# Which units' results stay in PSUM, where a softmax chunk ends, and GpSimd's order, in the first iteration of an attention and two-FFN kernel

## What is computed

```
w = exp(weight_gen - max) / (sum + 1e-9)              # softmax over the 7 taps
x1[b,s,h,g] = sum over k of w[b,s,h,k] * x[b,s-6+k,h,g]  # causal window of 7 tokens
h1 = x1 @ w_in1 ; g1 = h1 * cos(h1) ; x2 = g1 @ w_out1
h2 = x2 @ w_in2 ; g2 = max(0.01*h2, h2) ; out = g2 @ w_out2
```

## Time and profile before

| | |
|---|---|
| median of 3 executions | 1163.77 us |
| lowest and highest | 1163.77 and 1166.3 us |
| the profiled execution's own time | 1166.25 us |
| its span | 1164.4 us |
| TensorE matmul busy | 1146.1 us (98%) |
| VectorE, ScalarE, GpSimd busy | 900.9, 735.9, 84.9 us |
| granted TensorE clock, mean | 0.997 of full |

### The profile page before, as it was taken

The page is one execution under the profiler, slowest core; times in us unless marked ns, Lnnn a source line. Parts: engine busy times, 40 slices in busy tenths (PEclk is TensorE's granted clock), DMA queues, the critical chain, the costliest instruction groups (busy, mean ns, idle before and its releaser), DMA issues.

```text
span 1164.4 us, 23292 instructions
## 1 busy us (share of the span) xinstructions
PE 1146.1 (98%) x10170; PEld 950.1 (82%) x10170; DVE 900.9 (77%) x862; ACT 735.9 (63%) x804; POOL 84.9 (7%) x81
## 2 busy tenths in 40 slices
PE   7889999999999999999999999999999999999998
PEld 5768888888888888888888888888888888888876
DVE  8878797878879788697786868868697886968433
ACT  5666674766657676575755747566575655757554
POOL 5850000000000000000000000000000000000000
PEclk9999999999999999999999999999999999999999
DMA  9760101001010000101001010000101001000000
GB/s 260 202 120 1 35 1 49 1 2 49 1 49 1 20 30 1 49 1 49 1 2 48 1 48 1 22 28 1 48 2 49 1 1 48 1 15 1 15 1 28
DMA packets 20653, 37.40 MB, mean 32 GB/s; under 512 B 5196, under 2 KB 14794, under 8 KB 20168
## 3 DMA queue, kind: packets, MB, share of 16 engines
q1 hardware_dynamic: 16104, 30.66, 8.4%
q0 software_dynamic: 4448, 5.24, 2.5%
HBM read 29.61 MB, written 6.29 MB: 31 GB/s over the span
## 4 chain that ended last, share of the span: by engine, by line
PE 92%; DVE 2%; SPq 2%; POOL 2%; ACT 1%; issue 1%; DMA 1%; ACTq 0%; POOLq 0%
PE slot L1064 43%; PE acc_a L1064 28%; PE acc_b L1064 19%; DMA x_win<-in_x 1%; DVE g_lo L825 1%; POOL prods L307 1%; POOL prods L298 1%; SPq L463 0%; DVE prods L307 0%; POOL out_hi_lo L554 0%; PE slot L1009 0%; DVE gate L897 0%; PE acc_b L1037 0%; PE slot L996 0%; ACT g_hi L637 0%
## 5 line engine op out<-in xcount | busy, mean ns | idle before, releaser
L1064 PE MATMUL acc_a<-g_hi,out_hi_lo 64*128 64x512 f32 x2000 | 697.5, 389 | 0.0
L1064 PEld LDWEIGHTS acc_a<-g_hi,out_hi_lo 64*128 64x128 f32 x2000 | 369.0, 184 | 36.8
L825 DVE TENSOR_TENSOR g_lo<-gate,g_hi 128x1024 fp32r<-128x1024 f32 x248 | 303.6, 1224 | 117.5 <-ACT g_hi L637 116.9
L1064 PE MATMUL acc_b<-g_hi,out_hi_lo 64*128 64x512 f32 x1000 | 389.1, 389 | 1.6 <-DVE g_lo L825 1.5
L1064 PE MATMUL acc_b<-g_lo,out_hi_lo 64*128 64x512 f32 x1000 | 387.5, 387 | 0.0
L1064 PE MATMUL acc_a<-g_lo,out_hi_lo 64*128 64x512 f32 x1000 | 387.3, 387 | 0.0
L637 ACT ACTIVATE g_hi<-gate 128x1024 fp32r<-128x1024 f32 x248 | 262.9, 1060 | 94.3 <-PE acc_b L1064 77.5
L1064 PE MATMUL slot<-x_a_hi,in_a_lo 64*128 64x512 f32 x1024 | 299.6, 394 | 5.2 <-DVE g_lo L825 2.5
L1064 PE MATMUL slot<-x_b,in_b_hi 64*128 64x512 f32 x1024 | 296.4, 388 | 0.2 <-DVE x_b L839 0.2
L1064 PE MATMUL slot<-x_a_lo,in_a_hi 64*128 64x512 f32 x1024 | 296.3, 387 | 0.0
L1064 PE MATMUL slot<-x_a_hi,in_a_hi 64*128 64x512 f32 x1024 | 296.2, 387 | 0.0
(11 more groups left out here) (100 smaller groups left out, 1073.9 us busy)
## 6 DMA issues: line engine op xcount, KB each, us to landing
x_win<-in_x SPq DMA_DIRECT2D x14, 960.0 KB, 4.7
out<-result SPq DMA_DIRECT2D x16, 384.0 KB, 2.3
out_raw<-in_moe_w_out SPq DMA_DIRECT2D x3, 512.0 KB, 8.5
out_hi_lo<-in_moe_w_out POOLq DMA_DIRECT2D x2, 768.0 KB, 11.0
out_hi_lo<-in_moe_w_out POOLq DMA_DIRECT2D x1, 1536.0 KB, 14.5
taps_w<-in_weight_gen SPq DMA_DIRECT2D x2, 560.0 KB, 9.4
in_a_raw<-in_moe_w_in SPq DMA_DIRECT2D x1, 1024.0 KB, 5.3
out_raw<-in_moe_w_out SPq DMA_DIRECT2D x1, 1024.0 KB, 11.6
```

What stands on the lines that cost most here:

```text
L825: nc.vector.tensor_tensor(g_lo[:, q % 2, :], result_of(i - b, q), g_hi[:, q % 2, :].bitcast(FP32), ALU.subtract)\
L1064: return nc.tensor.matmul(to, w[rows, :], x[rows, :], start=start, stop=stop)
```

## The change

Three things change, all but one detail in iteration 0.

1. `stays` is true for units 2, 3 and 4 of iteration 0 alone. Units 0, 1, 5, 6 and 7 put their product into `gate`, and their slot is free once the product is done.
2. The softmax of chunks 1 and 2 keeps a common max, subtract and exp. The sum, guard, invert and multiply are done for chunk 1 alone ahead of unit 0, and for chunk 2 after step 9 of iteration 0, in half-size instructions. The load of the sine table moves from step 14 to 12.
3. GpSimd's `out_lows(2)` comes ahead of the first pair addition rather than behind it. VectorE's split of chunk 1's input comes after the fraction of unit 7, not ahead of it.

```diff
     def stays(i, q):
-        return i == 0 and q < len(FIRST_UNITS)
+        return i == 0 and q in (2, 3, 4)
...
-        SOFT_CHUNKS = [(0, 1), (1, 3), (3, 6), (6, 11), (11, C)]
+        SOFT_HEADS = [(0, 1), (1, 3), (3, 6), (6, 11), (11, C)]
+        SOFT_CHUNKS = [(0, 1), (1, 2), (2, 3), (3, 6), (6, 11), (11, C)]
...
-        EXP_STEP, SINE_STEP = 10, 14
+        EXP_STEP, SINE_STEP = 10, 12
...
+        SOFT_AT = {(0, 9): [(2, part) for part in TAIL_PARTS]}
...
             out_lows(1)
-            of_pool[2]()
             out_lows(2)
-            for instruction in of_pool[3:]:
+            for instruction in of_pool[2:]:
                 instruction()
...
-                if step == FIRST_INPUT_SPLIT and input_splits(i, step):
-                    split_low(FIRST_INPUT_STEP, i + 1)
                 if in_first and i == 0 and step == FIRST_UNITS[0]:
...
+                if step == FIRST_INPUT_SPLIT and input_splits(i, step):
+                    split_low(FIRST_INPUT_STEP, i + 1)
                 pending_low(i, step)
...
-                    if unit(j, UNITS.index(s)) == 0:
-                        pe.wait_ge(unit_dve, 3)
                     pe.wait_ge(lo_ready, unit(j, UNITS.index(s)) + 1)
                 elif what == "first":
+                    if unit(j, UNITS.index(s)) == 0:
+                        pe.wait_ge(unit_dve, 2)
                     pe.wait_ge(g_ready, first_units(j, UNITS.index(s)))
```

More of the change, by code:

```diff
@@ L275, in window_attention_two_ffn @@
         ATT_STEPS = 11
-        SOFT_CHUNKS = [(0, 1), (1, 3), (3, 6), (6, 11), (11, C)]
+        SOFT_HEADS = [(0, 1), (1, 3), (3, 6), (6, 11), (11, C)]
+        SOFT_CHUNKS = [(0, 1), (1, 2), (2, 3), (3, 6), (6, 11), (11, C)]
+        HEAD_OF = [n for a, _ in SOFT_CHUNKS for n, (b, e) in enumerate(SOFT_HEADS) if b <= a < e]
         ATT_MULTS = 9
-        SOFT_PARTS = ["max", "subtract", "sum", "guard", "invert", "multiply"]
-        SOFT_ORDER = [(n, part) for n in range(len(SOFT_CHUNKS)) for part in SOFT_PARTS]
+        HEAD_PARTS, TAIL_PARTS = ["max", "subtract"], ["sum", "guard", "invert", "multiply"]
+        SOFT_ORDER = []
+        for n, head in enumerate(HEAD_OF):
+            if head not in HEAD_OF[:n]:
+                SOFT_ORDER += [(head, part) for part in HEAD_PARTS]
+            SOFT_ORDER += [(n, part) for part in TAIL_PARTS]
         def soft_count(n, part):
@@ L399, in first_lows @@
                    b_pairs(W1.in_b_hi, cols).bitcast(FP32))
[L401 to L405 removed]
+        EXP_STEP, SINE_STEP = 10, 12
+        HEAD_ROWS, SOFT_ROWS = [[slice(a * J * heads, b * J * heads) for a, b in chunks]
+                                for chunks in (SOFT_HEADS, SOFT_CHUNKS)]
+        SOFT_AT = {(0, 9): [(2, part) for part in TAIL_PARTS]}
         for n, (begin, end) in enumerate(((1, 1), (2, 3), (4, 5)), 2):
@@ L408, in window_attention_two_ffn, with softmax_operands @@
             SOFT_AT.setdefault((begin, 8 if n == 2 else 14), []).append((n, "subtract"))
-            SOFT_AT[end, 13] = [(n, "sum")]
-            SOFT_AT[end, 14] = [(n, "guard"), (n, "invert")]
-            SOFT_AT[end, 16] = [(n, "multiply")]
+            SOFT_AT[end, 13] = [(n + 1, "sum")]
+            SOFT_AT[end, 14] = [(n + 1, "guard"), (n + 1, "invert")]
+            SOFT_AT[end, 16] = [(n + 1, "multiply")]
         EXP_AT, SINE_AT = [[(i, step) for i in (1, 3, 5)] for step in (EXP_STEP, SINE_STEP)]
-        def softmax_operands(n):
-            rows = SOFT_ROWS[n]
+        def softmax_operands(rows):
             part = taps_w[:, rows, :]
@@ L442, in load_gen @@
             def load_gen(n):
-                rows = SOFT_ROWS[n]
+                rows = HEAD_ROWS[n]
                 sp.dma_start(taps_w[:, rows, :], gen_rows[:, rows, :]).then_inc(gen_loaded[n], 16)
@@ L912, in step_of @@
                         dve.wait_ge(ready, n)
-                        nc.vector.scalar_tensor_tensor(slot[:, cols], slot[:, cols], RADIANS,
+                        nc.vector.scalar_tensor_tensor(result_of(i, q)[:, cols], slot[:, cols], RADIANS,
                                                        gate[:, 0, cols], ALU.mult, ALU.mult)\
@@ L934, in softmax @@
             def softmax(n, part):
-                rows = SOFT_ROWS[n]
+                rows = (HEAD_ROWS if part in HEAD_PARTS else SOFT_ROWS)[n]
                 weights, sums = taps_w[:, rows, :], scratch[:, rows]
@@ L941, in softmax @@
                     dve.wait_ge(soft, soft_count(n, "max"))
-                    ins = nc.vector.tensor_tensor(*softmax_operands(n), ALU.subtract)
+                    ins = nc.vector.tensor_tensor(*softmax_operands(rows), ALU.subtract)
                 elif part == "sum":
-                    dve.wait_ge(exp_ready, n + 1)
+                    dve.wait_ge(exp_ready, HEAD_OF[n] + 1)
                     ins = nc.vector.tensor_reduce(sums, weights, AX.X, ALU.add)
@@ L953, in softmax @@
                     dve.wait_ge(soft, soft_count(n, "invert"))
-                    ins = nc.vector.tensor_tensor(*softmax_operands(n), ALU.mult)
+                    ins = nc.vector.tensor_tensor(*softmax_operands(rows), ALU.mult)
                 ins.then_inc(soft, 1)
-            for part in SOFT_PARTS:
+            for part in HEAD_PARTS + TAIL_PARTS:
                 softmax(0, part)
@@ L963, in _ @@
                 nc.vector.tensor_tensor(lo, raw, hi, ALU.subtract).then_inc(w1_first_lo, 1)
-            for part in SOFT_PARTS[:2]:
+            for part in HEAD_PARTS:
                 softmax(1, part)
             split_low(INPUT_STEP, 0)
-            for part in SOFT_PARTS[2:]:
+            for part in TAIL_PARTS:
                 softmax(1, part)
```

8 lines of the change are left out of this document (4 added, 4 removed).

## The result

The changed kernel takes 1167.89 us (median of 11, 1166.77 to 1169.21) against 1165.14 us for the kernel before (11 runs, 1163.77 to 1166.58): ratio 1.0025, 95% interval 1.0016 to 1.0034. Timed again (run 1) it was 1167.91 against 1165.94 us, 1.002 (1.001 to 1.0029). So it is 2 to 3 us slower. The forecast was 1164.4 us and the range ended at 1167.3: missed.

A forecast was written before the change was run, and what follows sets the result against it. TensorE, busy 98% of the span, was taken as the bound, with only the first 80 us mattering. Terms +0.6 + 0.3 - 0.3 = +0.6 us on 1163.77 gave 1164.4 us, range 1159.3 to 1167.3.

The forecast's parts named there:

- the 0.3 us wait: TensorE's wait after 110 us, which loading the sine table at step 12 should take away: 0.3 us gained.
- the four waits: TensorE's waits of 2.38, 1.16, 2.48 and 1.23 us in the first 80 us; with slow stretches 10.7 us at most.
- Turns by whole instructions: VectorE and GpSimd: an instruction with two SBUF inputs waits for the other engine's running one, then precedes its next.
- rival 2: GpSimd's w_in2 instructions only stretch chunk 2's softmax tail, to 2.7 us in all: 1161.3 us, chance 0.25.
- Part 1: Fewer units stay in iteration 0: unit 0's fraction 1.06 us earlier; after its both_products the kernel 2.3 us ahead.
- GpSimd's chain: GpSimd's work from 29.72 us to chunk 1's attention: pair addition at 40.4, attention's end at 54.1, 0.4 us later.
- the reordering: out_lows(2) ahead of the first pair addition: would use 2.59 us of GpSimd idling, but VectorE's added turns eat it.
- part 2: Chunk 2's softmax tail after unit 7's low part: costs 5.1 us; iteration 1's first unit's sum 0.6 us behind.
- The rule on waits: TensorE: only waits over 2 us bring a slow stretch at 1.2 GHz, costing 1.7 us each.
- Rival 4: Held-up tail plus slow stretches behind unit 2's slot, unit 5's sum and the 2.5 us wait: 1167.8 us, chance 0.10.
- The base: The time before to which the forecast change of +0.6 us was added: the median, 1163.77 us, not the profiled 1166.25.

The follow-up runs named there:

- run 3: Changed kernel, but GpSimd starts its work on w_in2 only when the multiply of chunk 2's softmax is done: 1163.82 us, ratio 0.9989 to the kernel before.
- run 7: Changed kernel with out_lows(2) back behind the first pair addition and chunk 2's softmax tail after step 5 of iteration 1: 1164.49 us, ratio 0.9984.
- run 5: Changed kernel with 5 and 7 useless matmuls in TensorE's two waits ahead of the sum of iteration 1's first unit: 1166.24 us, ratio 0.9998.
- run 11: Kernel before with chunk 2's softmax ended after step 9 of iteration 0, sine table at step 12, split behind unit 7's fraction: 1164.23 us, ratio 0.9982.
- run 2: Changed kernel with chunk 2's softmax tail moved from after step 9 of iteration 0 to after step 5 of iteration 1: 1162.85 us, ratio 0.9978.

## Why the prediction was wrong

**What bounds the kernel.** Right: after 110 us nothing differs but the 0.3 us wait, which went as forecast (with it 0.5 us, counted from the fold on). One reading was wrong: the first of the four waits, which ends at 31.43 us with unit 0's low part, can't have the attention's end at 53.7 behind it; only the last three can.

**Turns by whole instructions.** Right, and run 3 shows it: 0.18 and 0.39 us against 1.97 and 2.13 with the same VectorE list. The rule of the Trainium skill (SBUF — State Buffer, Who interferes with whom) that the loser blocks for the full instruction is what the guard and the multiply do against instructions of 2.4 us, and the trace agrees: they end at 67.10 and 69.65 us, within 0.3 us of GpSimd's second and third instruction. The stretching of rival 2 would have made the tail 2.7 us long, and it was 4.9.

**Part 1 and GpSimd's chain.** The order of events was as worked out, at each step about 1 us earlier: pair addition 39.4 (forecast 40.4), attention's end 53.3 (54.1), unit 6's low part 61.2 (62.2), end of the tail 69.65 (70.9), the sum 76.56 (77.7). That VectorE's turns eat the reordering was half right: run 7 gives the order 1 us beside them. The 2.3 us by which the kernel was to be ahead were 3.0 (the first both_products of iteration 1 is over at 64.76 instead of 67.79), but they were worth nothing, since they only brought TensorE earlier to a wait whose end VectorE sets.

**The step that failed** is the last one of part 2: "so a slow stretch comes, but most of it lies under the wait for the low part; 0.3 us is left." It was 1.65 us in the first profile and 2.4 to 2.6 in the second, the median execution. The stretch did not begin with the fill after the first wait, as I had assumed, so that the second wait would cover it; it began at the end of the second wait (76.5 us) or within it (75.4), and nearly all of it fell on work. Runs 1 and 5 show its length and its price.

**The rule on waits** (only over 2 us) was too simple: two waits of 1.79 and 1.74 us with 1.4 us of work between them bring a stretch; a wait of 2.34 us has one behind it in the first profile of the changed kernel and none in the second. A pair of waits isn't needed either: single ones of 1.79 us (run 5) and 1.91 us (run 11, ahead of unit 3's fill) had a stretch behind them, and ones of 1.85 (run 3) and 1.87 us (run 11, ahead of the transpose) had none. So the length of the wait alone doesn't decide it, and what does is open. Rival 4 had the right mechanism for the last of its three stretches, at a price of 4 us in all and a chance of 0.10; of its other two, the one behind unit 2's slot never came and the one behind unit 5's sum came in one profile of two. A good part of it should have stood in the forecast.

**The base.** The time was forecast on the lowest of the three runs shown as median, though the profiled execution was 2.5 us above it. With 35 runs of before from 1163.37 to 1168.54 us (median 1165.94), a profile at 1166.25 is nearly the median, and the forecast should have been tied to it: 1166.85. That the first profiled execution of the changed kernel took just 1166.83 us would have been luck: its sum came 1.1 us earlier than forecast, and its stretch cost 1.3 us more.

## What to carry to other kernels

Before a cheap step is put into an engine's idle time, look at what the engine that it takes turns with (here GpSimd) does just then: an instruction of 0.2 us took 2 us, waiting for another's to end. And a wait removed early is worth nothing where a later one takes it in; worse, here it made the later ones long enough to bring half clock. Changes of which none costs anything alone (order -1.6 us; tail, with the earlier start, the moved split and the sine table, -2.3; part 1, with the moved split, none) came to +2.75 us together, so they have to be measured in combination too.

## What the runs showed of the hardware

TensorE's stretches at 1.2 GHz came in two lengths. The 14 profiled executions of this case hold 15 of them, all in the first 83 us: 11 lasted 3.4 us and 4 lasted 6.8 us, and the same kernel had both at the same place (76.5 to 79.9 and 75.4 to 82.2 us). The same wait of 2.34 to 2.35 us for unit 5's low part had a short one behind it (first profile of the changed kernel), none (runs 1 and 7) and a long one (run 2).

They are a large part of the run-to-run spread, as the mean granted clock of each execution shows. Of the 35 executions of the kernel before in the first group, 14 have a mean clock of 0.998 or more and a median of 1164.5 us, and 21 have 0.997 or less and a median of 1166.4; in the other two groups the difference is 2.0 and 2.1 us. What decides between none, the short and the long one is open: it wasn't tried.
